# Attention and two feed-forward stages on one core: the half swaps on ScalarE's queue, `y_slots` zeroed after routing, the first two pairs loaded and split side by side

## The reference

```python
# 4 x 8 heads, 576 positions, 64 per head; block-causal mask of 64
scores = q @ k.T / 8 ; attn = softmax(where(mask, scores, -1e9)) ; o = attn @ v
x = o as (2304, 512)
# routed feed-forward: 8 experts, 512 -> 1024 -> 512
do = x @ w_skip > 0 ; e = argmax(x @ w_gate) ; gate = softmax(...)[e]
x[do] += gate * (relu(x @ w1[e]) @ w2[e])
# dense feed-forward: 512 -> 2048 -> 512
h = x @ w_in ; out = (max(h, 0) + alpha * min(h, 0)) @ w_out
```

## Time and profile before

| | |
|---|---|
| median of 3 runs | 916.03 us (914.29 to 917.01) |
| the profiled execution | 918.93 us, of which 917.1 us are its span |
| busy in the span | PE 824.1 us (90%), PEld 724.6, DVE 431.3 (47%), ACT 264.6 (29%), POOL 241.0 (26%) |
| the chain that ended last | PE 74%; DMA 6%; SPq 6%; POOL 5%; issue 3%; DVE 3%; ACT 2% |
| queues | SP's q1 moves 74.50 MB, POOL's q0 15.73 MB, ACT's q10 12.58 MB |

### The profile page before, as it was taken

One profiled execution on the slowest core, in us unless ns is written; L12 is line 12 of the kernel. 1 busy time (PEld: TensorE's weight loads), 2 busy tenths in 40 slices (PEclk: granted clock), 3 DMA queues, 4 the chain that ended last, 5 costly groups with the idle time before them and its releaser, 6 DMA issues.

```text
span 917.1 us, 15528 instructions
## 1 busy us (share of the span) xinstructions
PE 824.1 (90%) x5243; PEld 724.6 (79%) x5244; DVE 431.3 (47%) x894; ACT 264.6 (29%) x642; POOL 241.0 (26%) x193
## 2 busy tenths in 40 slices
PE   5799999999802979999986999999999999999997
PEld 4578778888602969999965988898898998988996
DVE  2476766777751323222444464444444443453442
ACT  3556656666331212212221112112112112112111
POOL 4424243342054590330447871001001001000000
PEclk9899999999955989999996999999999999999999
DMA  5499999775225755532943312002002002000001
GB/s 117 85 268 243 263 245 253 205 192 142 75 91 182 269 204 206 168 107 91 331 160 103 104 47 69 0 0 69 0 0 69 0 0 69 0 0 35 1 1 34
DMA packets 97620, 103.06 MB, mean 112 GB/s; under 512 B 64320, under 2 KB 64320, under 8 KB 97088
## 3 DMA queue, kind: packets, MB, share of 16 engines
q1 hardware_dynamic: 89984, 74.50, 28.8%
q0 software_dynamic: 4448, 15.73, 5.3%
q10 hardware_dynamic: 3168, 12.58, 3.7%
HBM read 64.78 MB, written 27.53 MB: 101 GB/s over the span
## 4 chain that ended last, share of the span: by engine, by line
PE 74%; DMA 6%; SPq 6%; POOL 5%; issue 3%; DVE 3%; ACT 2%; ACTq 0%; DVEq 0%; POOLq 0%
PE bank L808 22%; PE bank L819 21%; PE bank L758 7%; PE bank L772 7%; PE bank L657 4%; PE bank L668 3%; PE bank L645 3%; DMA w_sb<-in_moe_w_dram 3%; POOL x_slots L529 2%; PE bank L621 2%; PE bank L691 2%; DMA q_t<-q_t 1%; POOL w_lo L552 1%; SPq L343 1%; PE bank L639 1%
## 5 line engine op out<-in xcount | busy, mean ns | idle before, releaser
L1252 DVE TENSOR_SCALAR g_sb<-bank,alpha_sb 128x384 f32<-128x384 f32 x96 | 59.3, 618 | 218.2 <-PE bank L808 217.7
L973 ACT CAST g_hi<-g_sb 128x384 fp32r<-128x384 f32 x96 | 49.4, 515 | 321.9 <-DVE g_sb L1254 321.9
L808 PE MATMUL bank<-u_hi,wi_hi 128*128 128x384 f32 x384 | 130.5, 340 | 1.4 <-DVE u_lo L1225 1.4
L808 PE MATMUL bank<-u_hi,wi_lo 128*128 128x384 f32 x384 | 130.3, 339 | 0.0
L808 PE MATMUL bank<-u_lo,wi_hi 128*128 128x384 f32 x384 | 129.9, 338 | 0.0
L819 PE MATMUL bank<-wo_lo,g_hi 128*128 128x512 f32 x288 | 113.7, 395 | 0.0
L819 PE MATMUL bank<-wo_hi,g_hi 128*128 128x512 f32 x288 | 112.8, 392 | 0.8 <-DVE g_lo L1258 0.8
L819 PE MATMUL bank<-wo_hi,g_lo 128*128 128x512 f32 x288 | 113.5, 394 | 0.0
L758 PEld LDWEIGHTS bank<-rows_t,w_sb 128*128 128x128 f32 x832 | 96.5, 195 | 2.6 <-DVE rows_t L1173 1.5
L758 PE MATMUL bank<-rows_t,w_sb 128*128 128x128 f32 x832 | 96.7, 278 | 1.1 <-DVE rows_t L1173 1.1
L864 ACT ACTIVATE p_sb<-bank,neg_max 128x128 f32<-128x128 f32 (+2 forms) x144 | 79.2, 552 | 59.1 <-DVE neg_max L1002 56.6
(11 more groups left out here) (147 smaller groups left out, 1280.7 us busy)
## 6 DMA issues: line engine op xcount, KB each, us to landing
w_sb<-in_moe_w_dram ACTq DMA_DIRECT2D x6, 2048.0 KB, 7.9
w_sb<-in_moe_w_dram SPq DMA_DIRECT2D x6, 2048.0 KB, 9.2
q_t<-q_t SPq DMA_DIRECT2D x64, 160.0 KB, 2.4
w_sb<-in_moe_w_dram SPq DMA_DIRECT2D x16, 512.0 KB, 6.2
x_slots<-x_tok SPq DMA_DIRECT2D x14, 512.0 KB, 3.3
y_slots<-x_tok SPq DMA_DIRECT2D x14, 512.0 KB, 5.0
qk_nat<-in_q_dram SPq DMA_DIRECT2D x32, 128.0 KB, 4.0
qk_nat<-in_k_dram SPq DMA_DIRECT2D x32, 128.0 KB, 3.6
```

The costliest lines, as they stand in the source:

```text
L808: last = pe.matmul(dst, w[:, j, P * f:P * f + P], u[:, j, :], start=z == 0, stop=z == len(terms) - 1)
L973: act.copy(g_hi[:, f % GB, :], g_sb[:, f % 2, :]).then_inc(g_hi_done, 1)
L1252: dve.tensor_scalar(g, a, 0.0, alpha_sb[:, f:f + 1], ALU.min, ALU.mult).then_inc(neg_done, 1)
```

## The change

1. **Swaps on ACT.** The transfers from `q_t` to `q_t` are issued by ACT and not by SP: the two of head 0 after the exponential of unit 5, the two of head 1 after the exponential of unit 7 and the last `qk_out` (`SWAP_AT = [5, 7]`). For pair 0 they follow its second and its fourth `qk_out`.
2. **Zeroing.** SP zeroes only `x_slots` in its rounds, from a buffer `zeros` of its own. `y_slots` is zeroed after `routed`, and only the tiles that no expert uses (from `tile_hi` of the last expert to 28), 128 rows a transfer. POOL waits for these (`y_zeroed`) before the gather. ACT no longer waits for `zeros_dma` before it copies the tails.
3. **The first pairs.** For pair 0 q is loaded by SP and k by ACT (`first_load`). Pair 1 is loaded right behind into `first_nat`, which lies where `p_t` will lie; before, it waited in `qk_nat` for the split of pair 0. The split of pair 0 is shared: DVE makes both parts of the q tiles and the remainder of the rest, ACT rounds the rest. TensorE starts when the first part is there (`first_split`). `load_qk(2)` waits for this split alone, and the small loads come right after it.

```diff
+        def first_load(queue, z, src):
+            for h in range(2):
+                queue.dma_start(qk_nat[:, FULL * z:FULL * z + FULL, h, :],
+                                src[h:h + 1, 0:MAIN, :].rearrange("a (t p) d -> p (a t) d", p=P)
+                                ).then_inc(first_loaded[z], 16)
+            queue.dma_start(qk_nat[TAIL * z:TAIL * z + TAIL, 2 * FULL, :, :],
+                            src[0:2, MAIN:S, :].rearrange("h p d -> p h d")).then_inc(first_loaded[z], 16)
...
                 if not isinstance(n, int):
-                    sp.wait_ge(split_done, n + 2)
-                    load_qk(n + 2)
+                    sp.wait_ge(split_done, n + 1)
+                    load_qk(n + 2, qk_nat, qk_loaded)
                 sp.wait_ge(pv_done, 2 * n)
                 load_v(n)
-                swap(n + 1)
-                for dst in (x_slots, y_slots):
-                    sp.dma_start(dst.rearrange("(t p) d -> p t d", p=P)[:, bass.ds(2 * n - 2, 2), :],
-                                 x_tok[:, T_TILES - 1:T_TILES, :].to_broadcast([P, 2, D])).then_inc(zeros_dma, 16)
+                sp.dma_start(x_slots.rearrange("(t p) d -> p t d", p=P)[:, bass.ds(2 * n - 2, 2), :],
+                             zeros[:].unsqueeze(1).to_broadcast([P, 2, D])).then_inc(zeros_dma, 16)
 
-            load_qk(0)
+            first_load(sp, 0, q_h)
+            load_qk(1, first_nat, second_loaded)
             sp.wait_ge(v_zero, 1)
             load_v(0)
-            sp.wait_ge(split_done, 1)
-            load_qk(1)
-            swap(0)
-            sp.wait_ge(split_done, 2)
-            load_qk(2)
-            swap(1)
+            sp.wait_ge(first_split, 2)
+            load_qk(2, qk_nat, qk_loaded)
...
             sp.wait_ge(routed, 1)
+            used = sp.value_load(tile_hi[0:1, E - 1:E], min_val=1, max_val=MAX_TILES)
+            with sp.Fori(used, SLOT_TILES) as g:
+                sp.dma_start(y_slots[bass.ds(g * P, P), :], zeros[:]).then_inc(y_zeroed, 16)
...
+            def swap(h, n, par):
+                act.wait_ge(qk_evac, QC * n + (2, 4)[h])
+                for to, at in ((0, DH), (DH, 0)):
+                    act.dma_start(q_t[to:to + DH, par, 1, h, :].bitcast(F32), q_t[at:at + DH, par, 0, h, :].bitcast(F32)
+                                  ).then_inc(swapped[h], 16)
...
                     for j, at in enumerate(QK_AT):
                         if at == c - 1 and not last:
                             qk_next(j, n, par)
-
+                    for h in range(2):
+                        if c == SWAP_AT[h] and not last:
+                            swap(h, n + 1, 1 - par)
+
+            first_load(act, 1, k_h)
+            act.wait_ge(ident_0, 1)
+            act.activation(warm[:], zero_c[:], ACT.Exp)
+            act.wait_ge(first_loaded[0], 48)
+            act.wait_ge(first_loaded[1], 48)
+            act.copy(parts[:, 0, FULL:, :, 0:DH], qk_nat[:, FULL:]).then_inc(first_hi, 1)
             act.wait_ge(const_ready, 1)
-            act.activation(warm[:], zero_c[:], ACT.Exp)
             for c in range(QC):
                 qk_out(c, 0, 0, RING[(c - QC) % 3])
+                if c in (1, 3):
+                    swap(c // 2, 0, 0)
...
-            for lo, hi in SPLITS:
-                dve.tensor_copy(to[:, lo:hi, 0:DH], nat[:, lo:hi]).then_inc(first_hi, 1)
-            for z, (lo, hi) in enumerate(SPLITS):
-                dve.wait_ge(first_hi, z + 1)
-                last = dve.tensor_tensor(to[:, lo:hi, DH:], nat[:, lo:hi], to[:, lo:hi, 0:DH].bitcast(F32), ALU.subtract)
-            last.then_inc(split_done, 1)
+            dve.wait_ge(first_loaded[0], 48)
+            dve.tensor_copy(parts[:, 0, 0:FULL, :, 0:DH], qk_nat[:, 0:FULL]).then_inc(first_copy, 1)
+            dve.wait_ge(first_copy, 1)
+            dve.tensor_tensor(parts[:, 0, 0:FULL, :, DH:], qk_nat[:, 0:FULL], parts[:, 0, 0:FULL, :, 0:DH].bitcast(F32),
+                              ALU.subtract).then_inc(first_split, 1)
+            dve.wait_ge(first_hi, 1)
+            dve.tensor_tensor(parts[:, 0, FULL:, :, DH:], qk_nat[:, FULL:], parts[:, 0, FULL:, :, 0:DH].bitcast(F32),
+                              ALU.subtract).then_inc(first_split, 1)
```

More of the change, by code:

```diff
@@ L88, in program @@
         START = (nc.sbuf_base + 63) // 64 * 64
-        sb = Region(START, nc.sbuf_usable_end)
+        ZEROS_AT = nc.sbuf_usable_end // 32 * 32 - 4 * D
+        zeros = Region(ZEROS_AT, nc.sbuf_usable_end)("zeros", [P, D], F32)
+        sb = Region(START, ZEROS_AT)
         x_tok = sb("x_tok", [P, T_TILES, D], F32)
@@ L99, in program @@
         tile_hi = sb("tile_hi", [1, E], I32)
+        tile_free = sb("tile_free", [1, 1], I32)
         alpha_sb = sb("alpha_sb", [P, FI], F32)
@@ L132, in program @@
         p_sb = sb("p_sb", [P, PB, QT * P], F32)
+        P_T_AT = sb.at
         p_t = sb("p_t", [P, 2, FULL, MAIN], F32)
+        first_nat = Region(P_T_AT, sb.at)("first_nat", [P, NAT, 2, DH], F32)
         p_tail_t = sb("p_tail_t", [P, QT, P], F32)
@@ L143, in program @@
         inv_sum = sb("inv_sum", [P, QT, 2], F32)
-        sb = Region(REST, nc.sbuf_usable_end)
+        sb = Region(REST, ZEROS_AT)
         wi_hi = sb("wi_hi", [P, KD, FD], F32R)
@@ L177, in program @@
         stage = sb("stage", [P, 1, FD], F32)
-        sb = Region(SMALL, nc.sbuf_usable_end)
+        sb = Region(SMALL, ZEROS_AT)
         u_sb = sb("u_sb", [P, CH, D], F32)
@@ L189, in program @@
         zeros_dma = sem("zeros_dma")
+        y_zeroed = sem("y_zeroed")
         w1_loaded = [sem("w1_loaded0"), sem("w1_loaded1")]
@@ L249, in program @@
         v_loaded = sem("v_loaded")
+        first_loaded = [sem("first_loaded_q"), sem("first_loaded_k")]
+        second_loaded = sem("second_loaded")
         first_hi = sem("first_hi")
+        first_copy = sem("first_copy")
+        first_split = sem("first_split")
         hi_done = sem("hi_done")
@@ L279, in program @@
         QK_AT = [2, 3, 3, 5, 6]
+        SWAP_AT = [5, 7]
         PV_AT, O_AT, SUMS_AT, ROWS_AT = 0, 2, 0, JOINT
@@ L332, in program, with load_qk @@
         MAX_TILES = SKIPPED // P
-        ZEROED = 16 * 2 * (PAIRS - 2)
+        ZEROED = 16 * (PAIRS - 2)
+        SLOT_TILES = MAX_TILES + 2
         W2Q = KF // KD
         assert MAX_TILES + 2 == 2 * (PAIRS - 2)
+        def first_load(queue, z, src):
[5 more added lines that the diff above has]
+                            src[0:2, MAIN:S, :].rearrange("h p d -> p h d")).then_inc(first_loaded[z], 16)
         @block.sync
         def _(sp):
-            def load_qk(n):
+            def load_qk(n, to, loaded):
                 for z, src in ((0, q_h), (1, k_h)):
                     for h in range(2):
-                        sp.dma_start(qk_nat[:, FULL * z:FULL * z + FULL, h, :],
+                        sp.dma_start(to[:, FULL * z:FULL * z + FULL, h, :],
                                      src[bass.ds(2 * n + h, 1), 0:MAIN, :].rearrange("a (t p) d -> p (a t) d", p=P)
-                                     ).then_inc(qk_loaded, 16)
-                    sp.dma_start(qk_nat[TAIL * z:TAIL * z + TAIL, 2 * FULL, :, :],
-                                 src[bass.ds(2 * n, 2), MAIN:S, :].rearrange("h p d -> p h d")).then_inc(qk_loaded, 16)
+                                     ).then_inc(loaded, 16)
+                    sp.dma_start(to[TAIL * z:TAIL * z + TAIL, 2 * FULL, :, :],
+                                 src[bass.ds(2 * n, 2), MAIN:S, :].rearrange("h p d -> p h d")).then_inc(loaded, 16)
             def load_v(n):
@@ L489, in split_pair @@
             def split_pair(n, par, first):
-                pool.wait_ge(qk_loaded, 96 * n + 96)
-                nat = qk_nat[:].rearrange("p t h d -> p (t h) d")
+                if first:
+                    pool.wait_ge(second_loaded, 96)
+                else:
+                    pool.wait_ge(qk_loaded, 96 * (n - 1))
+                nat = (first_nat if first else qk_nat)[:].rearrange("p t h d -> p (t h) d")
                 to = parts[:, par].rearrange("p t h d -> p (t h) d")
@@ L555, in _ @@
             last = pool.value_load(tile_hi[0:1, E - 1:E], min_val=1, max_val=MAX_TILES)
+            pool.wait_ge(back_ready, 1)
+            unused = pool.value_load(tile_free[0:1, 0:1], min_val=2, max_val=SLOT_TILES - 1)
+            pool.wait_ge(y_zeroed, 16 * unused)
             pool.wait_ge(y_stored, 16 * last + 32)
@@ L1006, in pt_out @@
                 dve.wait_ge(pt_tr, UNITS * n + c + 1)
-                if c == 0 and not first:
-                    dve.wait_ge(pv_done, 2 * n)
+                if c == 0:
+                    if first:
+                        dve.wait_ge(split_done, 1)
+                    else:
+                        dve.wait_ge(pv_done, 2 * n)
                 if c == JOINT:
```

22 lines of the change are left out of this document (4 added, 18 removed).

## The result

| | before | after |
|---|---|---|
| median | 916.12 us (914.29 to 917.01, 4 runs) | 972.54 us (967.97 to 974.48, 4 runs) |
| ratio | | 1.0613 [1.0577, 1.0648] |
| span of the profiled execution | 917.1 us | 972.6 us |
| mean granted clock | 0.958 | 0.945 |

The change makes the kernel 56 us slower. I had forecast 918.4 us, with a range to 928: it was wrong, and the term that failed is one that I had taken for a gain.

A forecast was written before the change was run, and what follows sets the result against it. It took TensorE as the bound in attention, other engines costing only its waits. Terms -3.3 - 6.35 - 4.5 + 16.6 = +2.4 us gave 918.4 us on the 916.03 median; range 905 to 928.

The forecast's parts named there:

- The late swaps: Eight attention pairs with weight loads: ACT issues swaps earlier, they land 2.66 us later, in time; 4.5 us gained.
- The rival that came true: Swaps in eight pairs land after 4.7 us, 1.2 us late each: 928 us; one of several cases sharing chance 0.24.
- my 57.1: Predicted time in us at which ACT issues the second of the first head's swaps in the pair shown.
- a need at 60.6: Predicted time in us at which TensorE needs the first head's swaps in the pair shown.
- the full wait for ACT: ACT's issue waits until the exponential in front has finished: 36 us lost, 936 us; one case sharing chance 0.24.
- ACT's issues: Swap issues at 0.57 us each delay attention's exponentials: 1.09 us a pair, 1.35 in pair 0, 16.6 us lost.
- The first rival: Issues hold ACT less, 0.41 us each: 6 us lost, about 908 us; 902 if exponentials aren't held; chance 0.28.
- The sum: All gains and losses together: +2.4 us on the profiled time, giving 918.4 us on the median.
- The start: First pair: split loads and split work start TensorE at about 6.35, scores right behind swaps landing at 11.75; 3.3 us gained.
- The wait for the small loads: Pair 0, before the tail products with v: small loads land before TensorE asks; 6.35 us gained.
- The zeroing: After attention: 15 transfers of 256 KB lie under the scatter, counted as nothing; up to 2 us if uncovered.
- Two queues that hold each other's issues: SP and ACT issuing together: first two issues wait 0.4 us each in eight pairs, 926 us; one case sharing chance 0.24.

The follow-up runs named there:

- experiment 3: The changed kernel, but SP sends zeroing, weights and the next q and k loads only after the next pair's swaps have landed; 923.77 us, one run.
- experiment 4: The changed kernel with swaps back on SP, issued behind each round's zeroing and weight loads; ACT issues none; 958.79 us, one run.
- experiment 1: The changed kernel with swaps issued by SP again, right behind the loads of v; new start and zeroing after routing stay; 905.40 us, ratio 0.9863.
- Experiment 6: The changed kernel with swaps back on SP and y_slots zeroed in the rounds again, leaving only the new start; 908.71 us, ratio 0.9897.
- experiment 5: The kernel before, swaps on SP, plus four small unused transfers a pair issued by ACT where the changed kernel issues swaps; 932.57 us, one run.
- experiment 2: The kernel before with only the swaps moved to ACT, old start and zeroing kept; 972.52 us, one run.
- experiment 7: The changed kernel, swaps on ACT, with the first two experts' weights loaded behind the last pair's v; 930.73 us, one run.

## Why the prediction was wrong

**The failed step** is "The late swaps": "landing 2.66 us later, as the first ones, they are in time ... 4.5 us gained". The issue came where I put it. The landing was priced from the first swap. In the old loop it was no longer (2.4 us, the line above), but there the swaps went out ahead of the bulk; in the new loop it is 8 to 9 us, with 1.5 MB sent just before. I read SP's lateness as a cost of the old order and did not see what the order gave: the swaps stood ahead of the bulk. ACT issues them by TensorE's progress, and SP, freed of the swaps, sends its bulk earlier, just ahead of them. Experiments 3 and 4 show this from both sides: the same issues on ACT with the bulk held back, 923.8 us; no issue on ACT and the bulk ahead, 958.8.

**The rival that came true was sized too small.** I did price a swap that lands late, at 4.7 us, the landing of the q and k loads, and got 928. Those loads did stand behind the bulk, but some way behind it: the first goes out at 64.56, 1.6 us behind the issue of the second weight load (62.95) and 3.8 behind that of the zeroing (60.77). The late swap goes out 0.35 us behind a weight load (58.29 against 57.94) and 1.6 behind the zeroing. The price left out how much of the bulk is still to be moved. An estimate from rows on record would have been: 1.5 MB at the 256 GB/s of the earlier trace rows are 6 us, the swap's own 2.66 come behind, and the bulk is 1 to 1.6 us ahead; that is 7 to 8 us. Behind my 57.1 it gives 64.1 to 65.1 against a need at 60.6: 3.5 to 4.5 us a pair, 28 to 36 us in eight, without the clock. (The 936 us of the full wait for ACT should have read 938: 36 in place of 16.6 on 918.4. Nothing hangs on it.)

**Not foreseen at all** was that such stands take TensorE's clock down: about 15 us in eight pairs.

**ACT's issues: right.** I took 0.57 us for one; they took 0.58 (median of 64). The exponential of unit 6 was to start 1.47 us behind the start of the copy; it started 1.48 behind it (187.20 to 188.68). The joint scores were to come 0.48 us late and did; a pair was to cost 1.09 us and cost 0.99. The kernel before had shown nothing of an issue on ACT beyond the one row of 0.41 us, so the 0.57 was a choice between that row and those of SP, and it hit. The first rival, that ACT would be held less, is out: the sentence of the Trainium skill that I cited for it (Advanced Engine Details and Errata, Sequencer Loop) is not borne out for what stands behind the issues, by the [0.43 <-issue] above; the exponential ahead of them did start, at 187.69, while the first one ran. Nor does the full wait for ACT's exponential occur: the first issue begins at 187.40, 0.29 us before that exponential does.

**The sum without the failed step** would have been 918.4 + 4.5 = 922.9 us; experiment 3, where swaps and bulk don't meet, measured 923.8. That it comes so near is luck: the product with v of pair 0 starts 4.6 us earlier than before (30.48) where the sum had 8.3, and the eight pairs take 4.8 us more than before (120.5 and 115.7) where the sum without the step had 8.7. The two misses cancel. The other seven are as summed, 6.7 us more against 6.5, and from the start of the last product with v to the end it is 2 us less.

**The start: half right.** The wait for the small loads is gone, as forecast. But TensorE starts at 7.31 and not 6.35, and the first scores stand at 14.30, where I had 11.8. The first part comes from loads that take 3.81 us to land and not 2.4; pair 1's loads now follow directly, which I didn't test as a cause. The second is the collision again, in small: after, the first swap takes 4.15 us beside `load_qk(2)`, while in experiment 1, where SP sends it ahead of those loads, the chain has

```profile
10.08 2.64 DMA q_t<-q_t
```

and the scores start at 12.85. Experiment 6 puts part 3 at 9.0 us on medians (8.1 by the start of the product with v of pair 0, 26.95 against 35.09), where I had 9.65.

**The zeroing: right.** It is issued from 319.35 us on, and lies under the scatter:

```profile
L439 SPq DMA_DIRECT2D y_slots<-zeros x15: 332/538/913, 319.3 to 333.8; - x15
```

SP's first load of rows follows only at 344.86, 26.3 us behind the first scatter (318.57); before it was 27.3. What follows attention is 1.9 us shorter than before.

**Two queues that hold each other's issues**, with which I priced 926, don't show at the very start, where SP and ACT issue side by side:

```profile
0.72 1.11 ACTq L353 DMA_DIRECT2D qk_nat<-in_k_dram  x2
...
0.73 1.01 SPq L353 DMA_DIRECT2D qk_nat<-in_q_dram  x2
```

Two issues take 1.0 to 1.1 us on each, as SP's next two do (1.12). It is otherwise with the first two swaps, which ACT issues while SP issues loads of v, q and k:

```profile
9.45 1.39 ACTq L874 DMA_DIRECT2D q_t<-q_t  x2
```

They take 1.39 us, and 1.12 in the quiet pair of experiment 3. With the long second issues of experiment 5 (up to 1.14 us) and experiment 2 (up to 1.39) this shows that something of the kind happens; what holds them stays open.

## What to carry to other kernels

A small transfer that somebody waits for is protected as long as its queue sends the bulk after it. Move it to another queue only if the bulk of the first stays behind it; ask what that queue will send in the microsecond before, and price the landing behind those bytes, not by a landing from an order in which it stood ahead of them. And count a stand of TensorE of several microseconds twice, since the work behind it may run at the lower clock.

## What the runs showed of the hardware

- A transfer of 160 KB landed 2.4 us after its issue (2.8 at most) when it was sent ahead of each round's bulk, with the transfer engines at 0.98. With 1.5 MB sent just before, those that TensorE waited for landed 5.7 to 8.0 us after it from the same queue and 7.9 to 9.0 from another.
- After stands of 4 to 5 us in each pair TensorE's granted clock was 0.50 (1.2 GHz) for some 3 to 6 us of full work, then 1.00 again. In experiment 7, whose waits in these pairs were 1.5 us at most, it was 1.00 throughout.
- ACT's issue of a swap started 0.00 to 0.20 us behind the start of the copy ahead of it (191.80 and 187.40 in experiment 3), beside the copy, and held only the exponential behind it. In the changed kernel SP's last issue of a round, the k load of the tails, took 2.5 us (median, 3.6 at most); that of the q load, three issues earlier, 0.64. What holds it wasn't tested.
